# Scores of two steps ahead set between the transpositions of the probabilities, in an attention and expert-routing kernel

## What is computed

```python
scores = scale * np.matmul(q, k.transpose(0, 1, 3, 2))
mask = (rel >= 0) & (rel < window)                       # window = 128
scores = np.where(mask, scores + bias[None], -1e9)
attn = np.exp(scores - scores.max(-1, keepdims=True))
attn = attn / (attn.sum(-1, keepdims=True) + 1e-9)
x = np.matmul(attn, v)             # then rows of 512, gate, top expert, two expert layers
```

## Time and profile before

| what | us |
|---|---|
| median of three runs | 466.28 |
| profiled execution, whole | 466.19 |
| its span in the profile | 464.2 |
| one round of the batch loop, from end of mix to end of mix | 40.07 |
| expert layers and what leads to them, from about 172 us on | 292 |

### The profile page before, as it was taken

How to read it: one execution, slowest core, us unless ns; L and a number is a source line. 1 busy time by engine, 2 the same in 40 slices (tenths; PEclk the granted TensorE clock), 3 DMA queues, 4 the chain that set the end, 5 groups by cost and what they waited for, 6 DMA issues and landing times.

```text
span 464.2 us, 11712 instructions
## 1 busy us (share of the span) xinstructions
PE 431.4 (93%) x2878; PEld 347.5 (75%) x2879; DVE 278.1 (60%) x804; ACT 217.1 (47%) x574; POOL 100.9 (22%) x156
## 2 busy tenths in 40 slices
PE   6999899989988898399999999999999999999982
PEld 5687678767766774288888888888888888888871
DVE  4678677767779887256266663663566666622330
ACT  3677678677765661144144451551555544211100
POOL 5190000000007831221112221222222222222111
PEclk9899999999999999799999999999999999999998
DMA  9995395168225027165166563463266666110110
GB/s 174 258 246 140 78 194 131 48 135 174 75 68 206 24 47 193 45 227 203 48 192 212 204 202 113 137 208 146 92 205 199 209 215 215 45 44 19 41 45 15
DMA packets 78856, 63.52 MB, mean 137 GB/s; under 512 B 61614, under 2 KB 61614, under 8 KB 78832
## 3 DMA queue, kind: packets, MB, share of 16 engines
q1 hardware_dynamic: 71504, 51.66, 40.6%
q0 software_dynamic: 3520, 10.76, 7.3%
q10 hardware_dynamic: 3808, 0.80, 1.1%
HBM read 53.77 MB, written 10.23 MB: 138 GB/s over the span
## 4 chain that ended last, share of the span: by engine, by line
PE 81%; DVE 7%; DMA 5%; issue 2%; SPq 2%; ACT 1%; POOL 0%; POOLq 0%; DVEq 0%
PE ps L1168 50%; PE ps L1009 7%; PE ps L1041 6%; PE ps L1052 5%; PE ps L1185 4%; PE ps L1022 4%; PE ps L987 3%; DVE probs L689 2%; PE ps L1161 2%; DMA x_rows<-x_sb 2%; DMA q_rows<-in_q 2%; DVE kT L701 1%; ACT qT L557 1%; DMA gathered<-x_rows,src_now 1%; SPq L356 1%
## 5 line engine op out<-in xcount | busy, mean ns | idle before, releaser
L1168 PE MATMUL ps<-weights_sb,rowsT_hi 128*128 (+1 forms) x336 | 106.6, 398 | 0.0
L1168 PE MATMUL ps<-weights_sb,hiddenT_hi 128*128 x336 | 103.5, 389 | 1.2 <-DVE hiddenT_lo L906 1.2
L627 ACT ACTIVATE hidden<-ps 128x512 f32<-128x512 f32 x21 | 12.5, 597 | 147.8 <-PE ps L1168 147.8
L925 DVE TENSOR_TENSOR weights_sb<-raw,weights_sb 128x1024 f32 (+1 forms) x56 | 67.1, 1220 | 15.9 <-issue 13.5
L1168 PEld LDWEIGHTS ps<-weights_sb,hiddenT_hi 128*128 128x128 f32 x336 | 63.0, 188 | 14.5 <-issue 1.4
L550 ACT ACTIVATE probs<-probs,mins 128x256 f32<-128x256 f32 (+2 forms) x160 | 73.7, 467 | 0.0
L1168 PEld LDWEIGHTS ps<-weights_sb,rowsT_hi 128*128 128x128 f32 x336 | 61.8, 189 | 12.7 <-issue 0.7
L1168 PE MATMUL ps<-weights_sb,rowsT_lo 128*128 (+1 forms) x168 | 65.8, 392 | 0.0
L1168 PE MATMUL ps<-weights_sb,hiddenT_lo 128*128 x168 | 65.4, 389 | 0.0
L906 DVE TENSOR_TENSOR hiddenT_lo<-ps,hiddenT_hi 128x512 fp32r<-128x512 f32 x42 | 27.0, 686 | 60.2 <-ACT hiddenT_hi L631 60.2
L616 ACT ACTIVATE weights_sb<-raw 128x1024 f32 (+1 forms) x56 | 56.5, 1065 | 4.8 <-DVE src_row L858 4.8
(11 more groups left out here) (126 smaller groups left out, 544.0 us busy)
## 6 DMA issues: line engine op xcount, KB each, us to landing
raw<-in_moe_w SPq DMA_DIRECT2D x64, 512.0 KB, 4.2
q_rows<-in_q SPq DMA_DIRECT2D x16, 256.0 KB, 4.7
v_rows<-in_v SPq DMA_DIRECT2D x16, 256.0 KB, 3.1
x_rows<-x_sb SPq DMA_DIRECT2D x16, 256.0 KB, 2.9
k_rows<-in_k SPq DMA_DIRECT2D x13, 256.0 KB, 5.0
k_rows<-in_k ACTq DMA_DIRECT2D x3, 256.0 KB, 5.7
q_rows<-in_q SPq DMA_DIRECT2D x4, 128.0 KB, 3.3
k_rows<-in_k SPq DMA_DIRECT2D x4, 128.0 KB, 3.3
```

The source lines that it names most:

```text
L925: vec.tensor_tensor(weights_sb[:, slot, 2 * layer + 1, part].rearrange("p s n -> p (s n)"), raw[:, j, :], weights_sb[:, slot, 2 * layer, p ...
L1168: ins = te.matmul(dst, left[a], right[c], start=first and n == 0, stop=last and n == 2)
```

## The change

`score` is taken apart: a new `score_pair(kk, n)` holds the two products of one n. `turn_probs` gets an argument `between`; if it is given, it sets `score_pair(between, odd)` behind its first transposition, so pair 0 stands in the even half and pair 1 in the odd half. In `batch` the waits for the operands of these scores go ahead of both halves, and the scores behind `turn_back` fall away, in all steps but the first of all and the last two of the last batch (37 of 40 steps). No instruction is added or taken away on any engine, other than in the register work of waits; VectorE's and ScalarE's orders stay as they are.

```diff
@@ score @@
                 for n in range(2):
+                    score_pair(kk, n)
+
+            def score_pair(kk, n):
+                i, quad = divmod(kk, 2)
+                if True:
                     for odd in range(2):
                         h = head(quad, 2 * odd + n)
...
-            def turn_probs(b, kk, odd):
+            def turn_probs(b, kk, odd, between=None):
...
                     for n in range(2):
+                        if between is not None and blk == 0 and n == 1:
+                            score_pair(between, odd)
                         at = (2 * blk + n) * P
...
-                    turn_probs(b, kk, 0)
-                    turn_probs(b, kk, 1)
+                    mixed_in = not (last and kk + 2 >= STEPS) and not (first and kk == 0)
+                    if mixed_in:
+                        nb, nk = b + (kk + 2) // STEPS, (kk + 2) % STEPS
+                        wait_alone(pe, qT_ready, nb * TI + nk // 2 + 1)
+                        wait_for_rows(nk // 2, kT_ready, nb * TI + nk // 2 + 1)
+                    for odd in range(2):
+                        turn_probs(b, kk, odd, nk if mixed_in else None)
...
-                    if not (last and kk + 2 >= STEPS):
+                    if not (last and kk + 2 >= STEPS) and not mixed_in:
                         score(b + (kk + 2) // STEPS, (kk + 2) % STEPS)
```

## The result

The changed kernel takes 482.14 us (median of four runs, 481.25 to 482.50) where the kernel before, timed beside it, takes 466.65. The ratio is 1.0324, with a 95% interval of 1.0298 to 1.0350. It is slower, by 15.5 us against the 14.0 forecast, inside the range of 475 to 486. The profiled execution took 481.25 us, with a span of 479.4.

The account below looks back on a forecast made before the run. TensorE was taken to bound the attention without a break. First batch +3.8, two loop rounds of +3.54 each and last batch +3.1 gave +14.0 us on the median of 466.28: 480.3 us, range 475 to 486.

Parts of the forecast that it names:

- Changes of shape: Between turn and mix, switching the part of TensorE's array in use costs 0.86 us a step against 0.36 before, +0.50.
- the rival by which the way back is cheap: Only the way into the scores costs: twice 0.15 less in 31 steps, 471.4 us; chance 0.08.
- The bare copy: Ahead of the mix, VectorE's odd-half copy is no longer covered, so the mix ends at 4.90, not 4.54: +0.36 us.
- The waits for q and k go: Ahead of turn-back, TensorE's waits for the copy of turned q or k are covered by the pairs: -0.19 us in the mean.
- Unit 4, no change between 64-row transpositions and scores: Unit 4's transpositions use 64 rows like the scores, so no change counted between them; two steps 6.86 us against 7.62.
- the first rival: Unit 4's crossings cost as much as the others: six steps, some 0.65 each, +4 us, 484.2; chance 0.17.
- Normalisation waited for at the next step's head: VectorE's late normalisation delays the next step's first turn by 0.1 us; unit 1's first step pays 0.3.
- the forecast's 43.61: One loop round, units 0 to 4, was to take 43.61 us against 40.07 before, +3.54 for each of two rounds.
- The rival with more waits than were counted: TensorE and VectorE pass work back and forth, each of 24 steps loses 0.3 more: +7, 487 us; chance 0.06.
- First batch +3.8: The first batch has nine changed steps, the missing one among those that gain: +3.8 us.
- Last batch +3.1: Last batch, VectorE-bound in its middle: step 3 -1.0, step 4 +1.5, steps 6 and 7 +1.6, others +0.8 and +0.2: +3.1 us.

Follow-up runs that it names:

- e3: The changed kernel with both pairs of scores behind the even half's first transposition, the odd half's copy still bare; 471.82 us, ratio 1.0060 to the kernel before.
- e4: The kernel before plus a small product on 64 rows behind each half's first transposition, steps 2 to 7 of each batch; 485.11 us, ratio 1.0304.
- e5: The kernel before plus the same small product as e4, but on all 128 rows, as control; 472.66 us, ratio 1.0082.
- e2: The changed kernel with the second pair of scores moved behind the odd half's last transposition; 472.00 us, ratio 1.0093 to the kernel before.
- e1: The kernel before with both pairs of scores whole behind the last transposition, ahead of turn-back, in the same 37 steps; 462.45 us, ratio 0.9871.
- e7: The changed kernel with VectorE's inverses of the sums made ahead of its copy of the odd half; 481.70 us, ratio 1.0266 to the kernel before.
- e6: As e1, but in step 4 of the last batch the scores stay behind the rank counts; 462.84 us, ratio 0.9851 to the kernel before.

## Why the prediction was right, point by point

- *Changes of shape, +0.50 a step of 256 keys*: right. The chain shows 0.63 and 0.49 where the sum has 0.63 and 0.48, e3 takes two changes away and gets 0.35 back, and e4 against e5 shows that it is the shape and no wait. The 0.49 also answers the rival by which the way back is cheap. In unit 2, where there was no wait to give back, the steps go from 3.99 (before) to 4.19 (e1), 4.54 (e2) and 4.85 (changed): 0.86 in all, the 0.50 and 0.36 of the sum.
- *The bare copy, +0.36*: right. The first load of the mix comes 0.04 behind the copy's end (estimated at 0.05), the copy is in the chain of every step of units 1 to 3, and e2 gets 0.32 back by covering it. The idle rows show 0.29 for it and not 0.36: the mix takes 1.09 from a standing start, and 1.02 right behind turn-back (e2's chain), which is the other 0.07. Idle time alone would have made the term too small.
- *The waits for q and k go, -0.19*: right. In the changed kernel no wait for L701 or L557 is left in TensorE's list, where the kernel before has 5.6 and 1.8 us. It goes in the last batch too.
- *Unit 4, no change between 64-row transpositions and scores*: right, 6.92 for its two steps against 6.86; the first rival needed some 8.2.
- *Normalisation waited for at the next step's head, 0.1 and once 0.3*: the mechanism was right, the size too small. It is 0.1 to 0.4 in unit 0's second step and the first steps of units 1 to 3, 0.84 in the second round. Two of these waits the profile doesn't put down to VectorE (0.20 and 0.11, ahead of units 2 and 3), but e7 takes them away. e7 makes it earlier in odd steps and gains 0.80 a round, which is the size of the miss of 0.8. That the round then comes to the forecast's 43.61 is luck in part: the forecast had counted some of this waiting in, and with e7 unit 0 still takes 0.22 more than forecast and unit 1 0.20 less. The rival with more waits than were counted had this mechanism, and counted 0.3 for each of 24 steps.
- *First batch +3.8*: 4.8, because one L707 took 1.37 us in step 3 and the normalisation behind it was waited for with 1.08 of idle time; the step behind takes 5.98 where it takes 5.09 in the loop. The sum had VectorE's work at its usual lengths. In the kernel before, a slow one of 1.12 two steps later was mostly hidden behind the scores and the mix (4.08 against 3.92 for the step behind it).
- *Last batch +3.1*: +3.7. Step 3 took 4.90 (4.9) and step 4 6.89 (6.9), with TensorE waiting for the ranks as said; the most of the miss is step 6, 4.57 against 4.16. The waits of step 4:

```profile
163.22 0.43 PE L987 MATMUL ps<-ident,q_rows 64*128 64x64 f32 x4 [0.72 <-DVE gate_part L727]
...
168.30 1.09 PE L1048 MATMUL ps<-probsT,v_rows 128*64 128x128 f32 x16 [1.08 <-DVE own_rank L767]
```

The steps together lost 4.81 + 4.25 + 4.32 + 3.73 = 17.1 us, 3.1 more than the sum. The total shows less because the first mix ended 1.3 us earlier than in the profile of before (14.92 against 16.26) and the stretch behind the attention was 0.6 shorter. The 1.3 us are the clock: behind a wait of 1.86 for the first blocks of q, the granted clock in the profile of before is at half from 12.95 to 16.36 us, and the scores of the first step take 2.08 us:

```profile
13.13 2.08 PE L1009 MATMUL ps<-kT,qT 64*128 64x256 f32 x8
```

In the profile of the changed kernel it is full there, behind a wait of 1.49, and the same scores take 1.14:

```profile
13.20 1.14 PE L1014 MATMUL ps<-kT,qT 64*128 64x256 f32 x8
```

The first mix ends at 16.0 to 16.3 in the profiles of before, e4 and e5 and at 15.75 in e6, all with the clock at half there, and at 14.4 to 14.9 in the other seven, with the clock full. Whether the change has a part in this, or only chance, isn't shown. So the steps in the profile were missed by 3.1 of 14, of which 0.9 is the one slow operation, and the total by 1.5; that the total is the nearer of the two is luck.

## What to carry to other kernels

Count the changes of TensorE's tile shape in a loop as if they were instructions, 0.10 to 0.20 us each here, and keep products of one shape together; filling a gap with products of another shape cost more here (0.35 for the way in and back) than the short gaps of 0.14 and 0.24 that it filled. Work that seems to stand idly between a producer's last output and its consumer may be the cover of another engine's copy: before moving it, set the copy's length against what is left. Where the work can go as a whole to the near side of a wait, with the cover kept, both are had: 1.3% faster here instead of 3.2% slower, for the same instructions. And read the granted clock behind long waits: behind several of 1.1 to 1.9 us it was at half here, and the products that followed took nearly twice as long.

## What the runs showed that was not expected

Single small VectorE operations in the batches that are written out take 0.7 to 2.4 us instead of their 0.16 to 0.3, and none in the loop. In step 3 of the last batch L707 is slow in all eleven profiles (0.94 to 2.23). In the first batch it varies: L707 in step 3 took 1.37 us in the changed kernel, 1.41 in its second profile and 2.35 in e6, but 0.16 in the kernel before, where another L707 further on (34.6 us) took 1.12, and in e1, e3 and e4 none there is slow. Here is the one of e6:

```profile
26.40 2.35 DVE L707 TENSOR_SCALAR sums_eps<-sums 128x8 f32<-128x8 f32 x1
```

The loop is spared in its first round as in its second, which speaks against something that is paid the first time a stretch of code is run. No run here tells what it is, and it stays open. One of them made the step behind it 1.6 us longer in e6 (5.82 against 4.19 in the loop). In the second profile of the changed kernel it brought a loss of clock too: behind the wait of 1.11 us that it caused, the granted clock is at half from 31.75 to 35.16 us, and the step takes 7.22 against 5.98.
